# A chunked-attention and two-MLP kernel on one core: one more prepared weight piece moves from GpSimd to ScalarE and VectorE

## The reference, cut to what matters

```python
# attention: batch 8, heads 8, 576 positions in 9 chunks of 64, head size 64
scores = q_c @ k_c^T / sqrt(64); attn = softmax(scores); x = attn @ v_c      # x: 4608 x 512
# first MLP (512 -> 1536 -> 512)
gate = 1 / (1 + exp(-(x @ w_gate))); x = (gate * (x @ w_val)) @ w_out
# second MLP (512 -> 2048 -> 512)
h = x @ w_in
g = where(h >= 1, h, where(h <= -1, 0, (h + 1)**2 / 4))
out = g @ w_out2
```

## Time and profile before

| | us |
|---|---|
| median of 3 runs | 1628.67 |
| lowest and highest | 1623.51, 1629.18 |
| the profiled execution | 1623.51 |
| its span in the trace | 1621.7 |
| PE busy | 1596.1 (98%) |
| DVE, ACT, POOL busy | 1133.7, 788.1, 513.7 |

### The profile page before, as it was taken

How to read it: one execution, slowest core, us unless ns; L and a number is a source line. 1 busy time by engine, 2 the same in 40 slices (tenths; PEclk the granted TensorE clock), 3 DMA queues, 4 the chain that set the end, 5 groups by cost and what they waited for, 6 DMA issues and landing times.

```text
span 1621.7 us, 29175 instructions
## 1 busy us (share of the span) xinstructions
PE 1596.1 (98%) x11176; PEld 1565.1 (97%) x11176; DVE 1133.7 (70%) x1611; ACT 788.1 (49%) x1269; POOL 513.7 (32%) x722
## 2 busy tenths in 40 slices
PE   8999999999999999999999999999999999999999
PEld 7899999999999999999999999999999999999998
DVE  4745667766695767678446579588578688588685
ACT  2323344434353444445334475575575575565663
POOL 7778844465675556566400000000000000000000
PEclk9999999999999999999999999999999999999999
DMA  9889899899899989988977877788788878778774
GB/s 295 293 283 342 279 362 357 311 339 364 326 339 356 351 322 339 372 321 324 333 282 265 281 298 277 258 298 284 256 296 284 276 294 273 283 293 258 259 280 169
DMA packets 135449, 489.50 MB, mean 302 GB/s; under 512 B 14224, under 2 KB 55696, under 8 KB 106256
## 3 DMA queue, kind: packets, MB, share of 16 engines
q1 hardware_dynamic: 106096, 417.24, 73.3%
q0 software_dynamic: 12032, 37.76, 6.0%
q10 hardware_dynamic: 17184, 32.64, 5.7%
HBM read 406.32 MB, written 81.26 MB: 301 GB/s over the span
## 4 chain that ended last, share of the span: by engine, by line
PE 85%; DVE 8%; DMA 3%; issue 2%; ACT 1%; ACTq 0%; DVEq 0%
PE banks L890 16%; PE banks L892 15%; PE banks L891 15%; PE banks L912 9%; PE banks L913 9%; PE banks L914 9%; DVE split_lo L1642 2%; PE banks L774 2%; PE banks L776 2%; DMA tile_in<-v_dram 2%; PE banks L775 2%; PE banks L744 1%; DMA ring<-w_in_split 1%; PE banks L765 1%; PE banks L753 1%
## 5 line engine op out<-in xcount | busy, mean ns | idle before, releaser
L890 PE MATMUL banks<-combo_hi,ring 128*128 128x384 f32 x1512 | 512.4, 339 | 3.5 <-DMA ring<-w_in_split 2.5
L892 PE MATMUL banks<-combo_hi,ring 128*128 128x384 f32 x1512 | 505.7, 334 | 0.0
L891 PE MATMUL banks<-combo_lo,ring 128*128 128x384 f32 x1512 | 505.3, 334 | 0.0
L912 PE MATMUL banks<-split_hi,ring 128*128 128x384 f32 x1092 | 366.8, 336 | 5.6 <-DVE split_lo L1642 5.0
L914 PE MATMUL banks<-split_hi,ring 128*128 128x384 f32 x1092 | 365.1, 334 | 0.0
L913 PE MATMUL banks<-split_lo,ring 128*128 128x384 f32 x1092 | 364.9, 334 | 0.0
L890 PEld LDWEIGHTS banks<-combo_hi,ring 128*128 128x128 f32 x1512 | 283.8, 188 | 6.9 <-DMA ring<-w_in_split 3.2
L891 PEld LDWEIGHTS banks<-combo_lo,ring 128*128 128x128 f32 x1512 | 284.0, 188 | 0.0
L892 PEld LDWEIGHTS banks<-combo_hi,ring 128*128 128x128 f32 x1512 | 283.8, 188 | 0.0
L1170 ACT ACTIVATE chain<-banks 128x384 f32<-128x384 f32 x324 | 157.4, 488 | 249.1 <-PE banks L892 247.9
L1642 DVE TENSOR_TENSOR split_lo<-g,split_hi 128x768 fp32r<-128x768 f32 x234 | 236.9, 1017 | 32.6 <-ACT split_hi L1247 31.2
(11 more groups left out here) (129 smaller groups left out, 2126.6 us busy)
## 6 DMA issues: line engine op xcount, KB each, us to landing
ring<-w_out_split SPq DMA_DIRECT2D x119, 1024.0 KB, 5.6
ring<-w_in_split SPq DMA_DIRECT2D x108, 1024.0 KB, 5.9
ring<-w_in_split SPq DMA_DIRECT2D x108, 768.0 KB, 7.9
ring<-w_out_split SPq DMA_DIRECT2D x35, 512.0 KB, 6.1
tile_in<-q_k_dram ACTq DMA_DIRECT2D x43, 384.0 KB, 6.6
w_in_split<-weights SPq DMA_DIRECT2D x36, 256.0 KB, 4.4
x_raw<-x_scratch SPq DMA_DIRECT2D x6, 1536.0 KB, 9.0
out_dram<-y SPq DMA_DIRECT2D x24, 384.0 KB, 6.3
```

The source lines that it names most:

```text
L890: pe.matmul(ps, w_lo, hi, start=first and k == 0, stop=False, skip_group_check=more)
L891: pe.matmul(ps, w_hi, lo, start=False, stop=False, skip_group_check=more)
L892: last = pe.matmul(ps, w_hi, hi, start=False, stop=k == 1, skip_group_check=more)
L912: pe.matmul(ps[:, j, :], w_lo, hi, start=first and k == 0, stop=False, skip_group_check=more)
```

## The change

Piece 10 moves from `POOLED` to `SIDE`: four pieces are prepared beside the tile stage instead of three, 16 side products instead of 12, and POOL prepares 14 pieces instead of 15, 56 products instead of 60.

The side products get other thirds. Before, products 0 to 7 had their difference in thirds 2, 4, ..., 16 and products 8 to 11 in 42, 45, 48, 51; the rounded copy came one third later, the remainder two and the store three thirds later. Now the differences are in thirds 4, 6, ..., 18, then 43, 45, 47, 49 and 53, 55, 57, 59; the rounded copy is in the same third, the remainder and the store in the next. The loads are issued in thirds 1, 2, 41 and 50 instead of ahead of third 0 and in 2 and 40; the fourth goes into the third one's buffer and waits for its last remainder. Two buffers for finished products, not three, serve products 0 to 7 (products 8 and up had two already), with two semaphores in all. POOL's wait of unit c = 8 for the side work falls; that of c = 9 for eight remainders stays, and the wait of c = 10 falls.

```diff
-SIDE = (0, 1, 11)
-POOLED = (2, 3, 4, 5, 6, 7, 8, 9, 10, 12, 13, 14, 15, 16, 17)
+SIDE = (0, 1, 10, 11)
+POOLED = (2, 3, 4, 5, 6, 7, 8, 9, 12, 13, 14, 15, 16, 17)
 def side_product(third):
-    if third % 2 == 0 and 2 <= third <= 16:
-        return (third - 2) // 2
-    if third % 3 == 0 and 42 <= third <= 51:
-        return 8 + (third - 42) // 3
+    if third % 2 == 0 and 4 <= third <= 18:
+        return (third - 4) // 2
+    if third % 2 and 43 <= third <= 49:
+        return 8 + (third - 43) // 2
+    if third % 2 and 53 <= third <= 59:
+        return 12 + (third - 53) // 2
     return None
...
             def side_buffer(n):
-            return side_early[n % 3] if n < 8 else side_late[n % 2]
+            return (side_early if n < 8 else side_late)[n % 2]
...
 # gpsimd, splitting the plain weights
-                    if n == 2 and c == 8:
-                        pool.wait_ge(side_split, 4)
                     if n == 2 and c == 9:
                         pool.wait_ge(side_split, 8)
-                    if n == 2 and c == 10:
-                        pool.wait_ge(side_stored[2], DMA * 2)
...
 # scalar
             def load_side(s):
                 if s < 2:
                     act.wait_ge(mixed_done, EARLY)
+                elif s == 2:
+                    act.wait_ge(x2_tile_stored, DMA)
                 else:
-                    act.wait_ge(x2_tile_stored, DMA)
+                    act.wait_ge(side_split, 4 * s)
...
-                        if third in (2, 40):
-                            load_side((2, 40).index(third) + 1)
-                        if side_product(third - 1) is not None:
-                            side_hi(side_product(third - 1))
-                        if side_product(third - 3) is not None:
-                            store_side(side_product(third - 3))
+                        if third in (1, 2, 41, 50):
+                            load_side((1, 2, 41, 50).index(third))
+                        if side_product(third) is not None:
+                            side_hi(side_product(third))
+                        if third and side_product(third - 1) is not None:
+                            store_side(side_product(third - 1))
...
 # vector
-                        if side_product(third - 2) is not None:
-                            side_lo(side_product(third - 2))
                         if side_product(third) is not None:
                             side_sum(side_product(third))
+                        if third and side_product(third - 1) is not None:
+                            side_lo(side_product(third - 1))
```

More of the change, by code:

```diff
@@ L216, in attention_and_mlps @@
         x2_tile = over(split_at, "x2_tile", [P, KT, N])
-        side_raws = [over(at, f"side_raw{b}", [P, 4, 2 * P]) for b, at in enumerate((5 * U, 3 * U, split_at))]
-        side_early = [over(b * U, f"side_early{b}", [P, U]) for b in range(3)]
+        side_raws = [over(at, f"side_raw{b}", [P, 4, 2 * P]) for b, at in enumerate((2 * U, 4 * U, split_at))]
+        side_early = [over(b * U, f"side_early{b}", [P, U]) for b in range(2)]
         side_late = [over(at, f"side_late{b}", [P, U]) for b, at in enumerate((split_at + 2 * U, x_at + 8 * N))]
@@ L247, in attention_and_mlps @@
         stage_ab = over(raw_at, "stage_ab", [P, 2, U])
-        assert 7 * U <= EARLY * EARLY_COLS and 3 * U <= KT * N and U <= 2 * N
+        assert 6 * U <= EARLY * EARLY_COLS and 3 * U <= KT * N and U <= 2 * N
         assert 30 * N + U <= OPERANDS_AT and chain_at + 8 * N + U <= x_at and 3 * N >= 2 * U
@@ L317, in side_raw @@
         def side_raw(n):
[L318 removed]
+            return side_raws[min(n // 4, 2)]
         def side_buffer(n):
[L321 to L325 removed]
+            return (side_early if n < 8 else side_late)[n % 2]
         def side_source(n):
@@ L353, in attention_and_mlps @@
         side_loaded = [sem(f"side_loaded{b}") for b in range(3)]
-        side_stored = [sem(f"side_stored{b}") for b in range(3)]
-        side_late_stored = [sem(f"side_late_stored{b}") for b in range(2)]
+        side_stored = [sem(f"side_stored{b}") for b in range(2)]
         ring_loaded = [sem(f"ring_loaded{b}") for b in range(RING)]
@@ L547, in load_ring @@
                     if piece in SIDE:
-                        for at in range(4 * SIDE.index(piece), 4 * SIDE.index(piece) + 4):
-                            done, used = side_signal(at)
-                            sp.wait_ge(done, DMA * (used + 1))
+                        for b in range(2):
+                            sp.wait_ge(side_stored[b], DMA * 2 * (SIDE.index(piece) + 1))
                     elif n < 2 * n_units(p) or n == 2 * n_units(p) + 4:
@@ L1107, in save_x2 @@
                     act.wait_ge(x2_tile_stored, DMA * t)
-                    act.wait_ge(side_split, 12)
-                    act.wait_ge(side_late_stored[0], DMA * 2)
+                    act.wait_ge(side_split, 16)
+                    act.wait_ge(side_stored[0], DMA * 8)
                 for j in (1, 3):
@@ L1123, in load_side @@
                     act.wait_ge(mixed_done, EARLY)
+                elif s == 2:
+                    act.wait_ge(x2_tile_stored, DMA)
                 else:
-                    act.wait_ge(x2_tile_stored, DMA)
+                    act.wait_ge(side_split, 4 * s)
                 four = pieces[SIDE[s], :, :, :].rearrange("b p n -> p b n")
-                act.dma_start(side_raws[s][:, :, :], four).then_inc(side_loaded[s], DMA)
+                act.dma_start(side_raws[min(s, 2)][:, :, :], four).then_inc(side_loaded[min(s, 2)], DMA)
             def side_hi(n):
                 act.wait_ge(side_summed, n + 1)
-                stored, used = side_signal(n)
-                if used:
-                    act.wait_ge(stored, DMA * used)
+                if n >= 2:
+                    act.wait_ge(side_stored[n % 2], DMA * (n // 2))
                 if n == 9:
@@ L1140, in store_side @@
                 place = operand_place(SIDE[n // 4], PREP_1[n % 4])
-                act.dma_start(place, side_buffer(n).rearrange("p (l n) -> p l n", l=2)).then_inc(side_signal(n)[0], DMA)
+                act.dma_start(place, side_buffer(n).rearrange("p (l n) -> p l n", l=2)).then_inc(side_stored[n % 2], DMA)
             def combo_part(p, k):
@@ L1474, in save_x2 @@
                     dve.wait_ge(x2_tile_stored, DMA * t)
-                    dve.wait_ge(side_late_stored[0], DMA * 2)
+                    dve.wait_ge(side_stored[0], DMA * 8)
                 for j in (0, 2):
@@ L1484, in side_sum @@
                 if n % 4 == 0:
-                    dve.wait_ge(side_loaded[n // 4], DMA)
+                    dve.wait_ge(side_loaded[min(n // 4, 2)], DMA * (2 if n == 12 else 1))
                 else:
@@ L1509, in x_sum @@
                     else:
-                        dve.wait_ge(side_late_stored[1], DMA * 2)
+                        dve.wait_ge(side_stored[1], DMA * 8)
                     dve.tensor_tensor(s, a22, a21, op=ALU.subtract).then_inc(combo_sum, 1)
```

3 lines of the change are left out of this document (1 added, 2 removed).

## The result

| | before | changed |
|---|---|---|
| median (5 runs each), us | 1626.57 | 1641.01 |
| lowest to highest | 1623.51 to 1629.18 | 1637.0 to 1642.15 |
| ratio, 95% interval | | 1.0085 (1.0065 to 1.0105) |
| span of the profiled execution | 1621.7 | 1635.0 |

The changed kernel is slower by 14.4 us, 0.85%; a second set of it gave 1.0062 (1.0041 to 1.0083). I forecast 6.4 us more and 1634. The time lies in the range of 1624 to 1643, but 0.85% is past the 0.5% that I gave a chance of 0.32, and 14.4 us is past the 8.1 from which I called the change clearly slower, with a chance of 0.2. (One reference in the prediction is misplaced: POOL's wait for a side remainder, 0.34 us, is in the earlier trace rows.)

The account below looks back on a forecast made before the run. PE, busy 98% of the span, was taken as the bound; its waits in the tile stage summed to 6.4 us more, 1629.9 on the profiled execution or 1635.1 on the median, so 1634 us was forecast, range 1624 to 1643.

Parts of the forecast that it names:

- POOL's relief gains nothing: POOL's first part ends earlier, but its 14.3 us idle wait for a matmul only grows: worth 0.
- POOL's unit of c = 9: Early tile stage: POOL's unit waits for the eighth side remainder, 3.8 us later than before; PE needs it only in third 29.
- ring load 4: Behind the tile stage: delayed 3.8 us against a margin of 2.7 us; taken as 0, up to 1.1 us lost.
- Third 58, +3.6: Round 14: late load 3 and side work delay ACT's copy of probabilities; PE waits 3.6 us more, 2.1 to 7.
- Thirds 22, 52 and 62: Rounds 7, 13, 15: shorter g_lo, -0.3 us; difference ahead of `normalize`, +0.3; remainder ahead of `shift` and difference behind, +0.7.
- Thirds 47 and 48, +1.0: Round 12, priced at third 48: side work and a store delay the copy of probabilities; +1.0 us, 0 to 2.
- Thirds 12, 13, 17 and 18, +1.1: Rounds 5 and 6: copy of probabilities later, +0.3 us at third 13 and +0.8 at third 18.
- the third rival: Clearly slower, 1642 us: side loads land late at thirds 8 and 58, long DVE instructions, about 13 us more; chance 0.2.

## Why the prediction was right or wrong

- **PE bounds, each wait in the stage reaches the end, POOL's relief gains nothing**: right. The rest of the span is 1424.0 us before and 1423.8 after (1427.0 in the second trace after, no more than in the traces of other kernels here). POOL's unit of c = 9 waited 4.3 us where 3.8 was worked out, and ring load 4 made no wait, since PE was later still.
- **Third 58, +3.6**: a wait of 3.53 us, by the chain that was written down. That the number fits is luck in part: load 3 took 5.1 us to land and not 6.1 (DVE waited 1.4 us for it), and the long difference and remainder (0.94 and 0.86 us, where I took 0.42) made up for it. These are two errors of opposite sign.
- **Thirds 22, 52 and 62**: -0.4, +0.35 and +0.7 for -0.3, +0.3 and +0.7. Third 53 had 0.35 us that I had not in the sum.
- **Thirds 47 and 48, +1.0**: 1.06 and 1.78 us, together 2.8. The difference of product 8 ahead of `shift` took 0.95 us, the product of `normalize` 0.93, the remainder of product 9 0.95: mis-sized, because the sum took the fast price for each, although the median in the earlier trace rows was 0.62. Here the page's rule on two-input VectorE instructions beside GpSimd (the Trainium skill, "SBUF — State Buffer", "Who interferes with whom") was the better guide; in all three places POOL's instructions lie beside them, and each is 0.4 to 0.5 us longer than at its shortest.
- **Thirds 12, 13, 17 and 18, +1.1**: in the first trace 0.9, 0.2 and 1.0 more for the first three and none for third 18; in the second, third 18 had 1.7. `normalize` was late in thirds 12 and 17, where I had counted as many side instructions ahead of it as before and put 0.
- **Third 67, not in the sum**: 0.66 us for a g_full that stood behind the sums of pass 0, which had waited 5.0 us for the store of a side product.
- **The missing term, +5.3**: the sum priced a wait at its own length. Behind some of them the clock was at half for 3.4 or 6.8 us, and PE's work in them took twice as long. In the kernel before no such stretch lies in the stage, so the profile of before showed none to ask about; its row of granted clocks is flat. But one of 3.4 us lies at 15.9 us, in the head, behind waits of PE of 1.2 and 1.4 us, and I did not read it. The trace of the changed kernel has none in the head.

Idle time, forecast at 6.4 us, was 9.9; the clock brought 5.3, forecast at 0; the earlier start gave back 1.9 in that trace, part of it the half clock of before's head.

Over many executions the clock counts for less than in this pair of traces. The record has the mean granted clock of each execution to three places. It was 0.9983 on average in 69 executions of the kernel before and 0.9969 in 14 of the changed one. Taken as lost time, that is 2.7 and 5.0 us, so by this estimate the clock brought 2.3 of the 11.2 us by which the average times differ (1627.9 and 1639.1), and waits about 9, against the 6.4 forecast. The clock also goes with the spread of one kernel: seven executions of before with a mean clock of 1.000 took 1623.3 us on average, 13 at 0.997 or less took 1631.2. The profiled execution of before, from which every term was read, was the fastest of the first five.

So the mechanism of the forecast was right and its sum too small: waits mis-sized by 3.5 us in this trace, and no term for the clock. That the time still lies in the range is owed to the range's width. It came near the 1642 of the third rival, but only half by that rival's road: DVE's instructions were long, but of the four loads only the last made DVE wait, 1.4 us.

## What to carry to other kernels

In a kernel that one engine bounds at 98%, ask of each instruction that moves what is queued behind it on its own engine, not only how long it runs: three DMA issues of 0.33 us, put one step later, brought the median down by 3.5 to 4.7 us here. Price a wait of PE at its own length plus the half-clock stretch that may follow, and price an instruction at its median beside its neighbours and not at its shortest. An engine's idle time before one wait is not its slack; look for every waiter on its last product.

## What the runs showed of the hardware that was not expected

- Behind waits of PE of 1.7 to 5.6 us the granted clock was at 0.50 for 3.4 or 6.8 us: 13 stretches in ten traces, not counting the head and the end of the span. The four of 6.8 us came behind the waits of 3.5 to 5.6 us. Behind others it stayed at 1.00: in 13 of 18 waits of 1.71 to 2.13 us, among them one of 1.8 at third 48 in the first trace of the changed kernel, where one of 1.9 at third 17 was followed by a fall; and behind two of 2.7 and 2.9 us, the latter in the run with two side pieces. No wait of 3.1 us or more was without a fall (five of them). What decides between the shorter ones was not settled.
- Behind waits filled with small matmuls, 28 records in 3.3 us and 60 in 6.8, the clock stayed at 1.00. These are two traces, and the waits would have been about 2.7 us long in both, a length behind which it did not always fall.
- The same DVE instruction of 128 x 256 took from 0.41 to 1.38 us within one execution.
